# First phase of an attention and MLP kernel: another order for VectorE and ScalarE, earlier loads, and weight pieces split by GpSimd alone

## What is computed

```python
for t in range(S):
    state = alpha[:, :, t, :, None] * state + np.einsum('bhd,bhe->bhde', k[:, :, t], v[:, :, t])
    y[:, :, t] = np.einsum('bhd,bhde->bhe', q[:, :, t], state)
```

```python
u = x + (xt @ U @ V).transpose(0, 2, 1)
x = u + np.maximum(u @ w_ch1, 0.0) @ w_ch2
h = np.maximum(x @ w_in, 0.0)            # 768x1024, halves u and v; v is normalised over its 512
out = (u * (w_spatial @ v_n + b_spatial)) @ w_out
```

## Time and profile before

| | |
|---|---|
| median of three runs | 759.46 us |
| the profiled execution | 759.09 us |
| its span | 757.3 us |
| TensorE, matmul | 715.5 us (94%) |
| VectorE | 347.4 us (46%) |
| ScalarE | 330.5 us (44%) |
| GpSimd | 202.4 us (27%) |

### The profile page before, as it was taken

One profiled execution on the slowest core, in us unless ns is written; L12 is line 12 of the kernel. 1 busy time (PEld: TensorE's weight loads), 2 busy tenths in 40 slices (PEclk: granted clock), 3 DMA queues, 4 the chain that ended last, 5 costly groups with the idle time before them and its releaser, 6 DMA issues.

```text
span 757.3 us, 25682 instructions
## 1 busy us (share of the span) xinstructions
PE 715.5 (94%) x11408; PEld 676.5 (89%) x11408; DVE 347.4 (46%) x607; ACT 330.5 (44%) x576; POOL 202.4 (27%) x141
## 2 busy tenths in 40 slices
PE   0588799999999999999999999999999999999998
PEld 0578698899999999999999899999998998999998
DVE  5897565545655455555553312115314322531531
ACT  3687556446436436446434422216133232422412
POOL 5420382120251120161120332221240150033031
PEclk9999899999999999999999999999999999999999
DMA  9404511121301031311000232221012002001001
GB/s 256 177 24 117 183 56 39 55 87 39 112 31 38 35 108 39 102 40 40 34 3 3 74 125 63 74 76 81 1 52 74 1 22 104 0 0 62 0 0 62
DMA packets 15692, 47.12 MB, mean 62 GB/s; under 512 B 1680, under 2 KB 8080, under 8 KB 15088
## 3 DMA queue, kind: packets, MB, share of 16 engines
q1 hardware_dynamic: 15600, 45.73, 18.9%
HBM read 36.29 MB, written 9.44 MB: 60 GB/s over the span
## 4 chain that ended last, share of the span: by engine, by line
PE 88%; ACT 3%; DVE 2%; issue 1%; DVEq 0%; ACTq 0%
PE HB L816 26%; PE ZB L816 9%; PE ZB L893 7%; PE ZB L895 7%; PE ZB L894 7%; PE SB L816 6%; PE SB L693 4%; PE ZB L929 3%; PE HB L929 3%; PE SB L798 2%; PE SB L929 2%; PE SB L807 2%; PE HB L934 2%; PE ZB L934 2%; PE SB L753 1%; PE SB L934 1%
## 5 line engine op out<-in xcount | busy, mean ns | idle before, releaser
L1403 DVE SCALAR_TENSOR_TENSOR hid_lo<-HB,hid_hi 128x384 fp32r<-128x384 f32 x96 | 53.5, 557 | 150.7 <-ACT hid_hi L1121 150.0
L1121 ACT ACTIVATE hid_hi<-HB 128x384 fp32r<-128x384 f32 x96 | 47.2, 492 | 159.5 <-PE HB L816 159.3
L816 PE MATMUL HB<-uh,w1h 128*128 128x384 f32 x288 | 103.8, 360 | 2.8 <-DVE ul L1399 2.8
L893 PE MATMUL ZB<-hid_hi,w2h 128*128 128x384 f32 x288 | 98.6, 342 | 0.0
L816 PE MATMUL HB<-ul,w1h 128*128 128x384 f32 x288 | 97.3, 338 | 0.0
L816 PE MATMUL HB<-uh,w1l 128*128 128x384 f32 x288 | 97.2, 337 | 0.0
L895 PE MATMUL ZB<-hid_lo,w2h 128*128 128x384 f32 x288 | 96.7, 336 | 0.0
L894 PE MATMUL ZB<-hid_hi,w2l 128*128 128x384 f32 x288 | 96.3, 334 | 0.0
L646 POOL TENSOR_TENSOR gl<-gated,gh 128x384 fp32r<-128x384 f32 x32 | 32.5, 1015 | 179.9 <-ACT gh L1136 179.9
L976 ACT COPY Qd<-Q 48x768 f32<-48x768 f32 x84 | 72.8, 867 | 17.7 <-PE SB L693 9.4
L615 POOL TENSOR_TENSOR Q<-Q,bk 112x768 f32<-112x768 f32 x14 | 26.0, 1857 | 176.2 <-ACT Qd L976 176.2
(11 more groups left out here) (227 smaller groups left out, 1473.2 us busy)
## 6 DMA issues: line engine op xcount, KB each, us to landing
Q<-in_q SPq DMA_DIRECT2D x8, 672.0 KB, 5.6
AL<-in_al SPq DMA_DIRECT2D x7, 672.0 KB, 4.7
K<-in_k SPq DMA_DIRECT2D x7, 672.0 KB, 4.7
Vt<-in_v SPq DMA_DIRECT2D x8, 576.0 KB, 3.8
mid<-x2s SPq DMA_DIRECT2D x8, 576.0 KB, 4.4
x<-mid SPq DMA_DIRECT2D x4, 1152.0 KB, 5.7
out<-o_sb SPq DMA_DIRECT2D x24, 192.0 KB, 1.8
x2s<-in_w SPq DMA_DIRECT2D x9, 384.0 KB, 3.9
```

What stands on the lines that cost most here:

```text
L816: last = nc.tensor.matmul(dst, weights(x, w), moving(y, m), start=(n == 0 and x == y == 0), stop=(n == total - 1 and y == 1))
L893: nc.tensor.matmul(bank, w2h[:, i, cols], hi, start=(i == 0), stop=False)
L1121: nc.scalar.activation(hid_hi[:, i % HID, :], HB[i % 2][:, 0:TILE], ACT.Relu).then_inc(h_hi, 1)
L1403: nc.vector.scalar_tensor_tensor(hid_lo[:, i % HID, :], HB[i % 2][:, 0:TILE], 0.0, hid_hi[:, i % HID, :].bitcast(F32), ALU.max, ALU.subtra ...
```

## The change

- Tables: the w1 pieces are split later, and in another order (the first half of every w1 row block first; `up` waits for the half that it reads).
- VectorE: the four first totals of a group come in one go ahead of Q; the other totals of group 1 ahead of its second take. `first_queries` serves level 2 too, for both groups, where GpSimd did it. The square copies stand together, behind level 6. Group 0's `kT` copies are VectorE's (`key_copies`). The queries of level 7 come behind the KV pieces. `att_start(1, 0)` comes behind the last u.
- ScalarE: the first spread of group 1 comes ahead of the copies of totals. Group 0's `kT` copies and the three w2 conversions are gone.
- GpSimd: `scale_q` begins at level 3. `split` makes the high part and the low part of pieces 6 to 8.
- SyncE: decay and keys of (1, 0) are loaded ahead of pieces 6 to 8, its queries and values behind them.

```diff
-HIGH1 = {(1, MASKED): [0], (0, LEVELS - 1): [1], (1, T_STEP): [2, 3], (1, KV_STEP): [4, 5]}
-LOW1 = {(0, LEVELS - 1): [0], (1, LEVELS - 1): [1], (0, AV_STEP): [2], (1, AV_STEP): [3], (0, AV_STEP + 1): [4],
-        (1, AV_STEP + 1): [5]}
-SPLIT_V = {(1, LEVELS - 1): [0, 1], (1, KV_STEP): [2]}
+HIGH1 = {(1, T_STEP): [0, 1], (0, KV_STEP): [2, 3], (0, Y_STEP - 1): [4], (1, Y_STEP - 1): [5]}
+LOW1 = {(1, KV_STEP): [0, 1, 2, 3], (1, AV_STEP + 1): [4], (1, AV_STEP + 2): [5]}
+SPLIT_V = {(1, LEVELS - 1): [0], (0, T_STEP): [1], (1, KV_STEP): [2]}
-SPLITS1 = {("xu", 0): [W1_PIECES], ("u", 0): [W1_PIECES + 1], ("u", 1): [W1_PIECES + 2]}
...
-        WEIGHTS1 = cut(w1, w1h, w1l, W1_PIECES) + cut(w2, w2h, w2l, W2_PIECES)
+        first = cut(w1, w1h, w1l, W1_PIECES)
+        WEIGHTS1 = first[0::2] + first[1::2] + cut(w2, w2h, w2l, W2_PIECES)
...
+            load_decay(1, 0, False)
+            sp.wait_ge(ld_al[0], 32)
+            load_keys(1, 0, False)
+            sp.wait_ge(ld_k[0], 32)
             for n in range(W1_PIECES, W1_PIECES + STAGE):
                 load_piece(n)
-            load_group(1, 0)
+            load_queries(1, 0, False)
+            sp.wait_ge(ld_q[0], 32)
+            load_values(1, 0)
+            sp.wait_ge(ld_v[0], 32)
...
+            def split(n):
+                where, loaded, value = slot(n)
+                pool.wait_ge(loaded, value)
+                _, hi, lo = WEIGHTS1[n]
+                nc.gpsimd.tensor_copy(hi, where).then_inc(w2_hi, 1)
+                pool.wait_ge(w2_hi, n - W1_PIECES + 1)
+                nc.gpsimd.tensor_tensor(lo, where, hi.bitcast(F32), ALU.subtract).then_inc(w_lo, 1)
...
-            for n in range(2, MASKED):
+            for n in range(3, MASKED):
                 for g in range(GROUPS):
                     scale_q(0, g, n)
             pool.wait_ge(w_lo, W1_PIECES)
             for n in range(W1_PIECES, W1_PIECES + STAGE):
-                split_low(n)
+                split(n)
...
-                if b == 0 and f == 0:
-                    pe.wait_ge(w_lo, W1_PIECES)
+                if b == t == 0 and i % (PIECE // P) == 0:
+                    pe.wait_ge(w_lo, (i * P // PIECE + 1) * W1_PIECES // 2)
...
-                if n == T_STEP:
+                if n == T_STEP and not (first and g == 0):
...
+            att_start(0, 0, True)
+            first_spread(0, 1)
+            att_start(0, 1, True)
             for g in range(GROUPS):
-                att_start(0, g, True)
-                first_spread(g, 1)
                 total_copies(g)
+            first_spread(1, 1)
...
-                    if b == 0:
-                        for n in SPLITS1.get((kind, i), []):
-                            split_high(n)
...
-                totals(0, g, [0])
+                totals(0, g, range(4))
                 dve.wait_ge(qd_ready[g], 2)
                 nc.vector.tensor_tensor(even(Q[g][:, :], 1), even(Q[g][:, :], 1), even(w.tot[1], 1), ALU.mult)
-                totals(0, g, range(1, 4))
...
+            def key_copies(g):
+                w = space(0, g)
+                for x, units in enumerate(T_BANKS):
+                    dve.wait_ge(aux_done[g], x + 1)
+                    nc.vector.tensor_copy(w.kT[:, units[0]:units[-1] + 1, :],
+                                          w.TB[x][:, 0:len(units) * ROWS].rearrange("p (u r) -> p u r", r=ROWS)
+                                          ).then_inc(aux_act[g], 1)
...
+                    if first and n == 2 and g == 0:
+                        first_queries(1, n)
                     scale_k(a, g, n)
...
             for n in range(1, MASKED):
                 for g in range(GROUPS):
+                    if (g, n) == (0, 2):
+                        first_queries(0, n)
                     for piece in range(vector_pieces(n)):
                         att_piece(0, g, n, piece, True)
-                    if (g, n) == (1, 1):
+                    if (g, n) == (0, 1):
                         totals(0, 1, range(4, LEVELS - 1))
             for g, n in LAST_STEPS:
-                if (g, n) == (0, MASKED):
-                    square_copies(0, QUARTERS[2:])
...
                 if (g, n) == (1, MASKED):
-                    square_copies(1, QUARTERS[2:])
-                if (g, n) == (1, LEVELS - 1):
                     for h in range(GROUPS):
-                        first_queries(h, n)
+                        square_copies(h, QUARTERS[2:])
+                if (g, n) == (0, T_STEP):
+                    key_copies(g)
+                if n == KV_STEP:
+                    first_queries(g, LEVELS - 1)
...
             for b in range(BATCH):
-                if b == 0:
-                    att_start(1, 0)
...
                     low(b, kind, i)
+                    if b == 0 and (kind, i) == ("u", NU - 1):
+                        att_start(1, 0)
```

More of the change, by code:

```diff
@@ L363, in build @@
         w_lo = sem("w_lo")
+        w2_hi = sem("w2_hi")
         al_used = [sem(f"al_used{g}") for g in range(GROUPS)]
@@ L616, in scale_q @@
                                         ).then_inc(q_ready[g], 1)
+            def split(n):
[5 more added lines that the diff above has]
+                nc.gpsimd.tensor_tensor(lo, where, hi.bitcast(F32), ALU.subtract).then_inc(w_lo, 1)
             def split_low(n):
-                pool.wait_ge(w_hi, n + 1)
+                pool.wait_ge(w_hi, n + 1 - STAGE)
                 _, hi, lo = (WEIGHTS1 + WEIGHTS2)[n]
@@ L1281, in first_queries @@
                 L = block_size(n)
-                dve.wait_ge(score_done[g], SCORES if n == LEVELS - 1 else n + 1)
+                if n < MASKED:
+                    dve.wait_ge(qd_ready[g], 2 * (n + 1))
+                else:
+                    dve.wait_ge(score_done[g], SCORES if n == LEVELS - 1 else n + 1)
+                dve.wait_ge(tot_ready[g], n - 1)
                 dve.wait_ge(q_ready[g], n - 1)
```

## The result

The changed kernel took 750.95 us in the median of four runs, against 759.56: a ratio of 0.9874 (95% interval 0.9847 to 0.9901). Run once more beside the kernel before, it gave 0.9891 (0.9871 to 0.9911). So the change gives about 8.5 us. I had forecast 4.45, and the low end of my range, 751.2, just missed the time. The profiled execution took 749.40 us, with a span of 747.6.

A forecast was written before the change was run, and what follows sets the result against it. TensorE's own work bounds the kernel after about 89 us, so gains count at the second scores of batch 1: 2.7 + 2.75 - 1.0 = 4.45 us off 759.46 gives 755.0, range 751.2 to 758.3.

The forecast's parts named there:

- step 5: Batch 1's totals beside GpSimd's new w2 chain, conversion taken as 1.3 us: second scores 2.75 us sooner, step 1 not included.
- step 6: Granted clock: short TensorE holes leave bound work at half clock, costing 1.0 us, bounds 0 and 2.
- Step 1: Opening, VectorE up to the fourth scores: totals no longer wait for GpSimd at the SBUF port, 2.7 us sooner.
- Step 2: Last steps of groups 0 and 1: conversions moved, key copies to VectorE, KV products 1.5 us sooner, bounds 1.1 and 1.6.
- Step 3: Mixing and u: totals behind u, w2 conversions off ScalarE; first up product 3.4 us sooner, step 2 included.
- Step 4: SyncE's load order: the 2.60 us wait for batch 1's keys goes, its first scores at 77.1 instead of 83.41.
- A: Rival: no port wait between batch 1's totals and GpSimd's chain, gain 7.5 us, 752.0; chance 0.2.
- B: Rival: GpSimd gets its turn first in the opening, or its conversion costs 1.8: 756.6, both 758.3; chance 0.2.
- C: Rival: gain taken back by holes in levels 2 to 7 of batch 1, 759; chance 0.07.
- D: Rival: slower through the new GpSimd chain, gain gone from 2.7 us a conversion, 763.9 at 4 us; chance 0.08.

The follow-up runs named there:

- one and a half: Changed kernel with the first half of each of GpSimd's three w2 conversions repeated, 1.3 us instead of 0.82: 753.63 us, ratio 0.9908 to the kernel before.
- three conversions: Changed kernel with GpSimd's conversion of each of the three w2 pieces made three times over: 756.27 us.
- late keys: Changed kernel with the keys of group 1 loaded behind one weight piece of 384 KB: 752.03 us against 750.67 for the changed kernel.
- ScalarE's order: Changed kernel with ScalarE's opening order (first spread of group 1, copies of totals) put back as before: 750.70 us.
- both waits: Changed kernel with GpSimd holding its third piece until batch 1's totals are made, and its x2s sums until VectorE's K: 751.23 us, ratio 0.9893.

## Why the prediction was wrong

**Direction, bound and path** were right. TensorE from the second scores of batch 1 on is nearly all of the kernel's length: 668.3 and 668.3 us before, 667.5 and 667.7 after. Of the 3.7 us by which the profiles beat the forecast, 2.0 arise up to the second scores (step 5) and 1.7 behind them (step 6).

**Step 1** was right in size (2.8 for 2.7) and in the turn at the port: K of group 1 took 1.17, and GpSimd waited. What I did not see is that its edits cover for each other, so that undoing one shows little.

**Step 2** was too high: 0.7 for 1.5. VectorE's key copies took 1.45, as reckoned, but they began late, behind square copies, K and a V split. My lower bound, 1.1, was for the copies' length and not for their start. The run with the copies back on ScalarE shows that this engine would have been ready sooner.

**Step 3** was near at the first up product (2.3 more for 1.9 more). The conversions were worth 1.3 to 1.6 of it, where I had 1.7; the rest is more than the 0.2 that I gave to the totals, but no run isolates it, and the two profiles of the kernel before differ by 0.9 here.

**Step 4** was right: 9.0 for 9.0 at the first scores (8.2 to 9.9 by single pairs of profiles), and the two runs on the load order confirm it from both sides. I gave it no weight in the sum, though, because I summed at the second scores. It is the part on which all the others hang: undone, the ratio is 0.9991.

**Step 5 is the step that failed.** From the first up product to the second scores I had 11.05 us and it was 9.05. "I take 1.3, the middle, as one input lies between none and two" is the sentence: the conversion is 0.82, close to the price of a pure write (0.7) and not to that of two inputs. The run with conversions of 1.3 us prices this at 0.9. The rest, 1.1, is the rule that each total waits out one more instruction, 3.3 us for each microsecond of conversion; with one and a half and with three conversions it cost less (0.9 and 3.7 us, where the rule gives 1.6 and 5.9), about 2 for each. The low-end figure that I had set beside it, 4.3 us sooner at 0.7 a conversion, was close to the 4.7 that came out (7.5 less 2.8 of step 1); by my own slope it should have read 4.7, so part of that closeness is luck. The Trainium skill (GPSIMD Engine Reference, 3.1) gives 1.8 cycles per element as the best case of a tight loop, against 2.6 with two inputs; from it I had estimated 1.15 us. It prices no conversion, and for the shortest loop bodies it has 1.03 cycles. The trace has 0.82 us, and the measurement decides.

**Step 6** had the wrong sign for this kernel. I took off 1.0; the changed kernel's granted clock stays at 1.00 from the first up product on, and behind the second scores its two profiles are 0.7 shorter instead. The likely place of most of it is the hole of 0.64 before the scores of level 6 in the trace of before, behind a K of 3.26; the K is 2.24 in the changed kernel and the hole is gone. But the change does not decide it. The run with level 2 on GpSimd has the changed program behind the second scores, and its VectorE shows

```profile
98.35 4.02 DVE L1249 TENSOR_TENSOR K<-K,small 112x768 f32<-112x768 f32 x1
```

with a hole of 1.45 and 668.2 us, as in the kernel before; four runs with other edits further ahead (late keys, ScalarE's order, conversions on ScalarE, three conversions) have 667.0 to 667.9, with that K at 2.2. The kernel before with ScalarE's new order has that K at 2.40, no hole ahead of level 6, and still 668.1. And the run in which GpSimd's sums wait for that K shortened it further and won nothing. So the cause of the 0.7 stays open, and it may be chance of the execution. The bounds of 0 and 2 for the clock were too narrow all the same: behind the second scores the run with conversions of 1.3 us has 672.1 us, the one with the third piece held back 670.2, against 667.5 and 667.7. Half a microsecond more of holes ahead of the second scores went with 2.6 to 4.5 more behind them in these two, but the runs with three conversions and with both waits, whose holes were as long or longer, have 667.1 and 667.7: in the first the half clock was nearly over at the second scores, in the second 3.4 us of it lay behind them and no hole followed.

**The rivals.** A (752.0) was nearest: little port waiting in step 5. B did not come: GpSimd got no turn first. C and D did not come. D's mechanism does occur, but its break-even lies further out: with 2.6 us for a conversion the ratio is still 0.996 (0.9939 to 0.9982).

## What to carry to other kernels

When several stages of a prologue wait for one another, price the change at the last mark that all of them meet, and undo each part by itself: here the load order alone brings 3 us of 8.5, all the rest alone nothing, and edits in the opening cover for each other. Bound a new instruction by its nearest kin, and weigh which kin it is; a one-input conversion on GpSimd was near a write and not half way to a two-input one. Before filling a hole on VectorE, look at what GpSimd does in it.

## What the hardware showed

- GpSimd: a conversion of 128x768 to fp32r took 0.82 us, half of it (128x384) 0.51, the two-input subtraction 1.83.
- VectorE with two SBUF inputs beside back-to-back GpSimd instructions: four small totals 4.34 us against 0.93 alone. By the Trainium skill (SBUF — State Buffer, Who interferes with whom) the one that issues first holds the port. The three totals of before agree. K of level 5 (0.95 us where GpSimd is idle) took 1.7 to 4.1 us in the profiles without a wait for it; where it took 4.02, from 98.35 to 102.37, GpSimd ended the instruction that it was in (99.64) and ran two more, to 101.56. So a VectorE instruction that has started can still be passed.
- The granted clock: holes of 1.1 and 1.6 us within 5 us left it at full in both profiles of the changed kernel; behind holes of 2.0 and 1.1 it was at half for 10 us, behind one of 3.2 for 7 in one run and 3 in another, behind one of 4.8 for 3. A single hole of 1.5 ahead of level 6 was followed by 3.4 us at half in one run (key copies on ScalarE) and by none in another (level 2 on GpSimd). So the length of a hole alone does not tell.
- The recorded clock and the durations don't always agree. The same 96 score matmuls took 1.51 us at a recorded 0.50 and 1.03 at 1.00 behind 80 us, but 1.51 at a recorded 1.00 at 33.02. So a recorded 1.00 in the first phase does not show that TensorE ran at 2.4 GHz there.
- The same first loads made the first scores of group 1 start at 16.3 to 19.9 us. In the changed kernel that goes through to the end (span less start 730.9 to 731.8 for starts of 16.7 to 19.9, the last with one more wait on GpSimd); in the kernel before, 0.8 of 2.4 us did.
